# Start-up of a complex linear-attention kernel: q and k side by side in memory, the decays formed later, and TensorE summing running products of two units

## Chip, core and metric

One core of a Trainium2 chip runs the whole program in one launch. The metric is the device time of one execution in microseconds (us), as the median of several runs.

## What is computed

Inputs have batch 4, 8 heads, 768 positions and head size 48. The first layer is a linear attention with a complex gate for each position and head dimension:

```
mag = sqrt(a_re^2 + a_im^2);  scale = min(mag, 0.999) / (mag + 1e-6);  a = scale * (a_re + i a_im)
S_t = a_t * S_(t-1) + k_t v_t^T        # S: 48 x 48, complex, one per head
y_t = q_t^T Re(S_t)
```

Its output (4 x 768 x 384) goes through a feed-forward layer (384 to 1024 and back, relu, a three-tap convolution over positions, a sigmoid gate), and then through a layer of four softmax attention experts of head size 64, of which each position takes two. All of it is fp32.

## The kernel before

A batch row is a stage of its own; the four rows run one after another (`main(b)` on each engine), and during a row's later stages the gates, q and k of the next row are prepared. The order of instructions on each engine is written out by hand, with semaphores between engines: an engine never reorders, so a wait holds everything behind it.

For the recurrence a row is cut into 6 chunks of 128 positions, and each chunk into two runs of 64 from its middle. W holds the running product of the gates of each run (`w_re`, `w_im`). The preparation works on three units of two chunks each, and goes through these steps:

- gates: square, magnitude, logarithm, exponential, three DVE steps (`norm`), `write_w`.
- running products (`cum`): a run of 64 is laid out as 8 groups of 8. Steps 0 to 6 multiply along one axis and steps 7 to 9 combine the last column by doubling, for all three units at once (`HEAD` = 10 steps, four DVE instructions each). Then one `cum_fill` for each unit multiplies the inner 7 x 7 of each run by its group's factor: three products (`cum_products`: re*re, im*im, re*im), and in `cum_combine` a subtraction, the fourth product and an addition, each waiting for the one before.
- 1/|W|^2: ACT squares both parts (`w_squares`), DVE adds them (`w_sumsq`), ACT takes ln and exp (`w_ln`, `w_guess`), DVE makes a Newton step of two instructions (`inverse`).
- q and k: two DVE instructions scale half of each (`scale_qk`), four products for each chunk multiply them by W (`products_by_chunk`, L1082 and L1085). SP stores the four to `qk_dram` (`store_first_chunk` for the first chunk of a unit, `store_unit` for the second; only row 0 stores chunks apart) and loads them back with heads in place of tiles (`load_heads`).
- `decay`: twelve DVE instructions on 15 columns form what carries the state from chunk to chunk; SP stores and reloads it.

After that, for each chunk c: TensorE transposes k (`transpose_k`, L1435), ACT copies it to `ktok` (`copy_k`, L638), TensorE makes the scores (L1448), the chunk's state gain (`gain`, L1460), the rotated state (L1472) and the outputs (L1497, L1499); DVE masks the scores (`mask`, L1093), adds the gain to the state (`state_sum`, L1108 for chunk 0 and L1111 after) and steps it (`state_step`, L1126 to L1131). `copy_x` (ACT) and `x_low` (DVE) write the chunk's output for the feed-forward layer, whose first products (L1513) for the second half of the positions wait for `x_low` of chunk 5.

Row 0 has nothing to hide its preparation behind. In this start-up TensorE also forms the low part of the first weight matrix (`w_in_rest`, L1422 and L1423: twelve matmuls of 512 columns into `wide[0]` to `wide[2]`; ACT takes them out with `w_in_low`, L629) and then runs three idle matmuls (`keep_busy`, L1415), before `transpose_k(0, 0)`. One fp32 matmul of 512 columns is two MATMUL records in the trace. The rest waits for `s_r0` of unit 0:

```
            pe.wait_ge(s_r0, 1)
            ...
            for k in range(KT):
                w_in_rest(k)
            keep_busy(HOLD)
            pe.wait_ge(s_winl, 1)
            transpose_k(0, 0, 0)
```

Of the kernel before, what the change touches and what calls it, by code (L numbers as in the profile page):

```python
# [40 lines left out]
P = 128  # L41
B, H, S, D = 4, 8, 768, 48
DM = H * D
# [39 lines left out]
HOLD = 3  # L83
LAST = B - 1
# [4 lines left out]
def program(nc, a_in, qk_in, v_in, w_in, conv_w, w_out, w_q, w_k, w_vg, w_o, consts, out, g_dram, qk_dram):  # L89
    with ExitStack() as ctx:  # L90
# [82 lines left out]
        qk_slot = heads[0:2 * D, :].rearrange("p (n x h t) -> p n x h t", n=SLOTS_A, x=2, h=H)  # L173
# [100 lines left out]
        s_gl = sem("decay_loaded")  # L274
        s_wsq = sem("w_squares")
# [74 lines left out]
        def k_of(c, hd):  # L350
            return qk_slot[:, c % SLOTS_A, 1, hd, :]

        def q_of(c, hd):
            return qk_slot[:, c % SLOTS_A, 0, hd, :]
# [16 lines left out]
        def cum_count(b, k):  # L371

            return b * (HEAD * HEAD_OPS + UNITS * FILL_OPS) + min(k, HEAD) * HEAD_OPS + max(k - HEAD, 0) * FILL_OPS
# [26 lines left out]

        def cum_fill(u):
# [6 lines left out]
            return ((lambda w: groups(w)[:, t, 0:WITHIN, 1:GROUP]),  # L410
                    (lambda w: groups(w)[:, t, WITHIN:GROUP, 0:WITHIN]
                     .broadcast_to([P, UNIT_RUNS, WITHIN, WITHIN])), temps)

# [16 lines left out]
        def _(sp):  # L430
# [33 lines left out]
            def store_unit(b, u):  # L464
# [3 lines left out]
                for n, (x, part, src) in enumerate(products):  # L468
                    sp.wait_ge(s_pr, 4 * (UNITS * b + u) + n + 1)
                    skip = 1 if b == 0 else 0  # L470
                    dst = qk_dram[x, part, UNIT_CHUNKS * u + skip:UNIT_CHUNKS * (u + 1)].rearrange("c (i p) t -> p (c i) t", p=P)
                    sp.dma_start(dst, tiles(src, u)[:, KT * skip:, :]).then_inc(s_sto[u], 16)

            def store_first_chunk(u):
# [3 lines left out]
                for n, (x, part, src) in enumerate(products):  # L478
                    sp.wait_ge(s_pr0, 4 * u + n + 1)
                    c = UNIT_CHUNKS * u  # L480
                    dst = qk_dram[x, part, c:c + 1].rearrange("c (i p) t -> p (c i) t", p=P)
# [104 lines left out]
        def _(act):  # L586
# [18 lines left out]

            def w_squares(b, u):

                act.wait_ge(s_cum, cum_done(b, u))
# [4 lines left out]
            def w_ln(b, u):  # L613
                act.wait_ge(s_n, UNITS * b + u + 1)
                nc.scalar.activation(m[:, 1, unit(u)], m[:, 0, unit(u)], ACT.Ln).then_inc(s_nl, 1)
# [129 lines left out]
            def main(b):  # L745
                more = b + 1 < B
                for c in range(NC):
# [7 lines left out]
                    if b == 0:  # L755
# [5 lines left out]
                        if c == 3:  # L761
                            guess(1, 0)
# [121 lines left out]
            nc.scalar.activation(negated[:], ident[:], ACT.Copy, scale=-1.0).then_inc(s_neg, 1)  # L884
# [951 lines left out]
```

## Time and profile before

| what | value |
|---|---|
| median of 3 runs | 757.24 us (754.28 to 763.18) |
| the profiled execution's own time | 751.82 us |
| its span on the core | 749.8 us |
| TensorE busy | 662.7 us (88%) |
| VectorE (DVE) busy | 614.0 us (82%) |
| ScalarE (ACT) busy | 410.4 us (55%) |
| mean granted TensorE clock | 0.998 |

The profiled execution took 2.0 us more than its span, and it lies 5.4 us below the median of the three timed runs: differences of a few microseconds between runs are of the size of the scatter. The rows of a timeline give the start in us, the duration in us, the engine, the line, the operation, what it writes and reads, its shape and its count; in brackets stand the engine's idle time before it and who ended it.

### The profile page before, as it was taken

What the parts mean: (1) busy time and instruction counts of PE and PEld (TensorE: products, weight loads), DVE (VectorE), ACT (ScalarE), POOL (GpSimd) and SP (SyncE); (2) the same over time, 40 slices, a digit from 0 to 9 for tenths busy, and PEclk for the clock granted to TensorE, in tenths of its full rate; (3) what the DMA queues carried; (4) which work ended last, traced back from release to release, by engine and by line L of the source; (5) the groups of instructions that cost most, each with busy time, mean ns of one, the idle gap of its engine ahead of it and who ended that gap; (6) DMA issues with size and microseconds to landing.
All of it is one profiled execution on the core that took longest, in us unless ns stands there. A gap on an engine that the chain in (4) does not pass through costs nothing.

```text
span 749.8 us, 13183 instructions
## 1 busy us (share of the span) xinstructions
PE 662.7 (88%) x5226; PEld 501.4 (67%) x5226; DVE 614.0 (82%) x1165; ACT 410.4 (55%) x747; POOL 0.2 (0%) x4
## 2 busy tenths in 40 slices
PE   0006989999999999999999999999999999999998
PEld 0002768776666788776566788776566888998765
DVE  3999998999999787998989787998988675773663
ACT  6404367434667656335668647335667335654565
POOL 0000000000000000000000000000000000000000
PEclk9999999999999999999999999999999999999999
DMA  8704785200049464100058464100055440000001
GB/s 342 270 0 119 203 244 189 93 0 1 0 121 271 121 181 159 61 0 1 0 142 258 124 175 167 48 1 0 1 147 170 131 128 2 1 0 1 2 22 43
DMA packets 93628, 73.84 MB, mean 98 GB/s; under 512 B 8704, under 2 KB 85760, under 8 KB 92928
## 3 DMA queue, kind: packets, MB, share of 16 engines
q1 hardware_dynamic: 93568, 73.01, 32.1%
q8 instruction: 41, 0.67, 0.4%
q14 instruction: 19, 0.16, 0.1%
HBM read 49.34 MB, written 23.65 MB: 97 GB/s over the span
## 4 chain that ended last, share of the span: by engine, by line
PE 53%; DVE 32%; ACT 7%; issue 3%; DMA 3%; SPq 0%; DVEq 0%; ACTq 0%
DVE cv L1138 6%; PE wide L1603 6%; PE wide L1448 5%; PE wide L1584 5%; PE bank L1655 4%; PE wide L1639 4%; PE bank L1663 4%; PE wide L1460 3%; PE wide L1513 3%; DVE m L956 3%; PE wide L1534 3%; DVE heads L1143 3%; PE wide L1579 2%; DVE m L955 2%; PE wide L1575 2%
## 5 line engine op out<-in xcount | busy, mean ns | idle before, releaser
L1513 PE MATMUL wide<-x_hi_lo,win_hi 128*128 128x384 f32 x384 | 107.7, 350 | 3.4 <-DVE x_hi_lo L1102 2.6
L1513 PEld LDWEIGHTS wide<-x_hi_lo,win_hi 128*128 128x128 f32 x384 | 69.8, 188 | 7.7 <-issue 4.6
L1534 PE MATMUL wide<-heads,wout 128*128 128x384 f32 x200 | 70.1, 494 | 4.8 <-DVE heads L1143 4.8
L1202 DVE TENSOR_REDUCE nmax<-wide 128x1 f32<-128x768 f32 (+2 forms) x96 | 55.3, 618 | 21.1 <-PE wide L1613 21.0
L1138 DVE SCALAR_TENSOR_TENSOR cv<-h,wconv,cv 128x768 f32<-128x768 f32 x64 | 64.9, 1014 | 9.0 <-ACT cv L681 7.4
L1603 PE MATMUL wide<-attn 64*128 64x512 f32 (+3 forms) x256 | 65.0, 482 | 2.3 <-ACT attn L705 2.3
L1513 PE MATMUL wide<-x_hi_lo,win_lo 128*128 128x384 f32 x192 | 64.5, 336 | 0.0
L729 ACT ACTIVATE xs<-wide 128x896 f32<-128x896 f32 x48 | 44.1, 918 | 37.1 <-PE wide L1639 37.1
L655 ACT ACTIVATE h<-wide 128x384 f32<-128x384 f32 x64 | 29.6, 490 | 56.0 <-PE wide L1513 29.2
L1422 PE MATMUL wide<-attn,ident 128*128 128x512 f32 x4 | 3.9, 1082 | 62.3 <-ACT m L620 62.3
L1534 PEld LDWEIGHTS wide<-heads,wout 128*128 128x128 f32 x200 | 36.6, 189 | 30.5 <-DVE heads L1143 10.3
L686 ACT ACTIVATE cv<-cv 128x768 f32<-128x768 f32 x32 | 27.1, 846 | 48.6 <-DVE cv L1138 48.4
L1448 PE MATMUL wide<-heads 96*128 96x128 f32 x384 | 49.4, 283 | 3.8 <-DMA heads<-heads_dram 2.1
L1448 PEld LDWEIGHTS wide<-heads 96*128 96x128 f32 x384 | 45.6, 194 | 8.1 <-issue 4.1
L1655 PE MATMUL bank<-xs,attn 128*64 128x128 f32 x672 | 46.4, 279 | 0.2 <-ACT xs L729 0.2
L1655 PEld LDWEIGHTS bank<-xs,attn 128*64 128x64 f32 x672 | 35.8, 136 | 13.5 <-ACT xs L729 8.1
L1422 PEld LDWEIGHTS wide<-attn,ident 128*128 128x128 f32 x4 | 1.2, 323 | 63.3 <-issue 63.3
L1603 PEld LDWEIGHTS wide<-attn 64*128 64x128 f32 x256 | 25.5, 184 | 24.1 <-issue 9.3
L720 ACT ACTIVATE cv<-wide,nmax 128x768 f32<-128x768 f32 (+2 forms) x48 | 38.0, 792 | 2.9 <-DVE nmax L1202 2.5
L1093 DVE TENSOR_TENSOR attn<-wide,cmask 128x512 f32<-128x512 f32 x48 | 31.0, 682 | 9.6 <-PE wide L1448 9.6
L1639 PE MATMUL wide<-ident,cv 128*128 128x128 f32 x240 | 34.9, 276 | 3.5 <-DVE cv L1217 2.3
L1513 PEld LDWEIGHTS wide<-x_hi_lo,win_lo 128*128 128x128 f32 x192 | 36.1, 188 | 2.0
(205 smaller groups left out, 1505.1 us busy)
## 6 DMA issues: line engine op xcount, KB each, us to landing
heads<-heads_dram SPq DMA_DIRECT2D x96, 192.0 KB, 3.6
araw<-a_in SPq DMA_DIRECT2D x12, 768.0 KB, 6.2
araw<-qk_in SPq DMA_DIRECT2D x12, 768.0 KB, 4.7
heads_dram<-m SPq DMA_DIRECT2D x18, 384.0 KB, 3.6
heads_dram<-araw SPq DMA_DIRECT2D x18, 384.0 KB, 2.9
v<-v_in SPq DMA_DIRECT2D x4, 1536.0 KB, 6.7
out_dram<-h SPq DMA_DIRECT2D x24, 192.0 KB, 2.1
heads_dram<-m SPq DMA_DIRECT2D x12, 192.0 KB, 2.8
```

What stands on the lines that cost most here:

```text
L720: nc.scalar.activation(prob[side][:, t % 2, 0:n], slot_scores(t, side), ACT.Exp, bias=nmax[:, t, side:side + 1], accum_out=zsum[:, t, side ...
L729: nc.scalar.activation(probT[:, t % PROBT, :], wide[2][:, 0:KEYS], ACT.Copy).then_inc(s_pc, 1)
L1093: TT(sc[:, c % 2, 4 * quad:4 * quad + 4, :], low[2 + quad].rearrange("p (h t) -> p h t", h=4), cmask[:].unsqueeze(1).broadcast_to([P, 4, P ...
L1138: STT(cb, hb[:, tap:tap + S], wconv[:, mt, tap:tap + 1], cb, ALU.mult, ALU.add).then_inc(s_c, 1)
L1202: dve.tensor_reduce(nmax[:, t, side:side + 1], slot_scores(t, side), AXX, ALU.max, negate=True).then_inc(s_nm, 1)
L1448: last = MM(low[2 + quad][:, hh * P:(hh + 1) * P], k_of(c, hd), q_of(c, hd), start=True, stop=True)
L1513: last = MM(low[u % 2][:, 0:NT], w[:, k, mt * P:(mt + 1) * P], xs[:, k, n * NT:(n + 1) * NT], start=(k == 0 and part == 0), stop=(k == KT ...
L1534: last = MM(mlp_bank[u][:, 0:NT], wout[:, mt, k * P:(k + 1) * P], hgate(mt)[:, n * NT:(n + 1) * NT], start=(mt == 0), stop=(mt == MT - 1))
L1584: last = MM(bank_u[:, 0:NT], w[:, k, i * P:(i + 1) * P], xT[:, k, n * NT:(n + 1) * NT], start=(k == 0), stop=(k == KT - 1))
L1603: MM(slot_scores(t, side)[:, lo:hi], qT[rows, e // 2, i * P:(i + 1) * P], kT[rows, e // 2, lo:hi], start=True, stop=hi != keys(t, side))
L1639: last = nc.tensor.transpose(dst[:, j * P:(j + 1) * P], prob[side][:, t % 2, j * P:(j + 1) * P], ident[:])
L1655: last = MM(out_bank[side][rows, o:o + P], vx[:, j, e * HD:(e + 1) * HD], probT[:, (t + r) % PROBT, span(t, side)][:, j * P:(j + 1) * P], ...
```

## The change

Four things are changed.

1. `qk_dram` is laid out (part, chunk, row, q or k, position) in place of (q or k, part, chunk, row, position), and `heads` likewise, so that q and k of a row are 1024 bytes side by side. A `load_heads` then issues two DMAs of 384 KB in place of four of 192 KB; stores are as many as before and write runs of 512 bytes, 1024 bytes apart.
2. In row 0, units 1 and 2 are filled in another way. DVE makes all four products and no sum (`summed_product`; the fourth goes to `xs`), TensorE adds them with identity matmuls in PSUM (`fill_sums`), ACT copies the two sums into W (`fill_copy`). The sum of squares of unit 1 is also made by TensorE (`w_sums`), and read from PSUM by `w_ln` and `inverse_first`. TensorE starts `w_in_rest` after seven steps of `cum` and not after unit 0's exponential.
3. In row 0, `decay` runs right after the products of chunk 0, and its store stands before `store_unit(0, 0)` on SP.
4. In row 0, the ACT table load and `ln(1, 0)` for the next row move from behind `copy_x(0, 2)` to behind `copy_k(0, 4)`.

The order on ACT, DVE, TensorE and SP in the start-up, with the new functions (parts left out are marked):

```diff
-        qk_slot = heads[0:2 * D, :].rearrange("p (n x h t) -> p n x h t", n=SLOTS_A, x=2, h=H)
+        qk_slot = heads[0:2 * D, :].rearrange("p (n h x t) -> p n h x t", n=SLOTS_A, h=H, x=2)
...
-                for x in range(2):
-                    for part in range(2):
-                        sp.dma_start(qk_slot[part * D:(part + 1) * D, c % SLOTS_A, x, :, :],
-                                     qk_dram[x, part, c].rearrange("(h d) t -> d h t", d=D)).then_inc(s_hd[c % SLOTS_A], 16)
+                for part in range(2):
+                    sp.dma_start(qk_slot[part * D:(part + 1) * D, c % SLOTS_A].rearrange("p h x t -> p h (x t)"),
+                                 qk_dram[part, c].rearrange("(h d) x t -> d h (x t)", d=D)).then_inc(s_hd[c % SLOTS_A], 16)
...
             store_first_chunk(0)
+            store_decay(0)
             store_unit(0, 0)
             load_heads(0, 0)
             load_heads(0, 1)
-            store_decay(0)
             load_decay(0)
...
+            def fill_copy(u, part):
+                act.wait_ge(s_fm, 4 * (u - 1) + part + 3)
+                act.wait_ge(s_fs, 2 * (u - 1) + part + 1)
+                nc.scalar.activation(fill_of((w_re, w_im)[part], u),
+                                     fill_sum(part).rearrange("p n (i g) -> p n i g", g=WITHIN),
+                                     ACT.Copy).then_inc(s_fc, 1)
...
                         if c == 3:
+                            exp_tables()
+                            ln(1, 0)
                             guess(1, 0)
...
                         if c == 2:
                             magnitude(1, 1)
-                            exp_tables()
-                            ln(1, 0)
...
+            w_in_low(0)
             w_squares(0, 0)
+            w_in_low(1)
             w_ln(0, 0)
             w_guess(0, 0)
+            w_in_low(2)
+            for part in range(2):
+                fill_copy(1, part)
             w_squares(0, 1)
-            w_in_low(0)
             w_ln(0, 1)
             w_guess(0, 1)
-            w_in_low(1)
-            w_in_low(2)
+            for part in range(2):
+                fill_copy(2, part)
+            w_squares(0, 2)
             copy_k(0, 0)
-            w_squares(0, 2)
...
             cum(0, 0, HEAD + 1)
-            for u in range(2):
-                cum_products(0, HEAD + 1 + u)
-                w_sumsq(0, u)
-                cum_combine(0, HEAD + 1 + u)
-                if u == 1:
-                    decay(0)
-                inverse(0, u)
-                scale_qk(0, u)
-                products_by_chunk(u, 0)
-                if u == 1:
-                    w_sumsq(0, UNITS - 1)
-                    mask(0, 0)
-                    state_sum(0, 0)
-                products_by_chunk(u, 1)
+            for n in range(3):
+                summed_product(1, n)
+            w_sumsq(0, 0)
+            summed_product(1, 3)
+            for n in range(2):
+                summed_product(2, n)
+            inverse(0, 0)
+            scale_qk(0, 0)
+            products_by_chunk(0, 0)
+            decay(0)
+            for n in range(2, 4):
+                summed_product(2, n)
+            products_by_chunk(0, 1)
+            inverse(0, 1)
+            scale_qk(0, 1)
+            dve.wait_ge(s_fc, 2)
+            products_by_chunk(1, 0)
+            w_sumsq(0, UNITS - 1)
+            mask(0, 0)
+            state_sum(0, 0)
+            products_by_chunk(1, 1)
...
+            def fill_sums(u):
+                planes_of = ((m[:, 0, unit(u)], ident, m[:, 1, unit(u)], negated),
+                             (m[:, 2, unit(u)], ident, fill_extra(u), ident))
+                for part, (one, one_by, other, other_by) in enumerate(planes_of):
...
+                    pe.wait_ge(s_fm, 4 * (u - 1) + 2 * part + 2)
+                    for runs_of in (slice(0, GROUP), slice(GROUP, UNIT_RUNS)):
+                        cols = slice(runs_of.start * fill_size, runs_of.stop * fill_size)
+                        MM(fill_sum(part)[:, runs_of, :], one_by[:], one[:, cols], start=True, stop=False)
+                        last = MM(fill_sum(part)[:, runs_of, :], other_by[:], other[:, cols], start=False, stop=True)
+                    last.then_inc(s_fs, 1)
+            def w_sums():
+                pe.wait_ge(s_winl, KT)
+                pe.wait_ge(s_wsq, SUMMED[0] + 1)
...
-            pe.wait_ge(s_r0, 1)
+            pe.wait_ge(s_cum, cum_count(0, WITHIN))
             pe.wait_ge(s_neg, 1)
             pe.wait_ge(s_winh, KT)
             for k in range(KT):
                 w_in_rest(k)
+            fill_sums(1)
+            w_sums()
+            fill_sums(2)
             keep_busy(HOLD)
-            pe.wait_ge(s_winl, 1)
+            pe.wait_ge(s_fc, 4)
             transpose_k(0, 0, 0)
             transpose_k(0, 0, 1)
-            pe.wait_ge(s_winl, 2)
             scores(0, 0)
             pe.wait_ge(s_cast, 2)
-            pe.wait_ge(s_winl, KT)
+            pe.wait_ge(s_rn, 2 * SUMMED[0] + 1)
             gain(0, 0)
```

`fill_size` is 49, so a part of `fill_sums` has 588 columns, each multiplied twice; `w_sums` has 768 columns, each multiplied twice.

## Rows read from the trace of the kernel before

**Rows 1.** The page, part 4: the chain that ended last, by engine.

```profile
PE 53%; DVE 32%; ACT 7%; issue 3%; DMA 3%; SPq 0%; DVEq 0%; ACTq 0%
```

**Rows 2.** Busy time by stage: stretch, length, PE, PEld, DVE, ACT, POOL, PEclk, DMA, GB/s.

```profile
125.00:200.00 75.00, 72.26 (x296) 53.90 (x297) 70.53 (x117) 38.41 (x65) 0.00 (x0) 1.00 0.14 48
```

**Rows 3.** Waits for a DMA between 250 and 330 us: total, times, longest.

```profile
PEld wide L1448 <- DMA heads<-heads_dram: 0.2, 1, 0.2
```

**Rows 4.** Timeline of DVE in the start-up.

```profile
47.48 0.68 DVE L955 TENSOR_TENSOR m<-W 128x504 f32<-128x504 f32 x1
...
57.46 0.77 DVE L959 TENSOR_TENSOR m<-W 128x588 f32<-128x588 f32 x1
...
59.51 0.95 DVE L1031 TENSOR_TENSOR m<-m 128x768 f32<-128x768 f32 x1
60.38 0.77 DVE L973 TENSOR_TENSOR W<-m 128x588 f32<-128x588 f32 x1
...
62.67 0.95 DVE L1037 TENSOR_TENSOR m<-m 128x768 f32<-128x768 f32 x1
...
75.12 0.18 DVE L1008 TENSOR_TENSOR lf<-W,first 128x15 f32<-128x15 f32 x1
...
76.78 0.96 DVE L1037 TENSOR_TENSOR m<-m 128x768 f32<-128x768 f32 x1
...
84.43 1.02 DVE L1082 TENSOR_TENSOR m<-araw,W 128x384 f32<-128x384 f32 x2
...
88.62 0.55 DVE L1129 TENSOR_TENSOR st<-bank,gcol 96x384 f32<-96x384 f32 x1 [0.45 <-PE bank L1472]
...
90.47 0.55 DVE L1111 TENSOR_TENSOR attn<-wide,st 96x384 f32<-96x384 f32 x1 [0.70 <-PE wide L1460]
```

**Rows 5.** Timeline of TensorE, start-up and the scores of chunk 4.

```profile
62.32 2.04 PE L1422 MATMUL wide<-attn,ident 128*128 128x512 f32 x2 [62.32 <-ACT m L620]
...
75.29 2.74 PE L1415 MATMUL bank<-attn,ident 128*128 128x512 f32 x6
77.86 0.83 PE L1435 MATMUL wide<-ident,heads 96*128 96x96 f32 x8
...
80.34 1.48 PE L1460 MATMUL wide<-v,cv 128*96 128x48 f32 x16
...
83.60 2.84 PE L1448 MATMUL wide<-heads 96*128 96x128 f32 x16 [1.78 <-DVE attn L1093]
...
106.97 2.05 PE L1448 MATMUL wide<-heads 96*128 96x128 f32 x16 [1.13 <-DMA heads<-heads_dram]
```

**Rows 6.** Timeline of ACT in the start-up.

```profile
57.46 1.49 ACT L609 ACTIVATE m<-W 128x1536 f32<-128x1536 f32 x1 [28.98 <-DVE W L977]
...
68.62 1.03 ACT L629 ACTIVATE win_lo<-wide 128x1024 fp32r<-128x1024 f32 x1 [4.35 <-PE wide L1423]
```

**Rows 7.** Timeline of SP's queue: the loads of chunks 0 and 1, and of chunk 4.

```profile
70.86 4.21 SPq L495 DMA_DIRECT2D heads<-heads_dram  x8
...
101.61 1.87 SPq L495 DMA_DIRECT2D heads<-heads_dram  x4
```

**Rows 8.** The page, part 6: DMA issues, KB each, median us from issue to landing.

```profile
heads<-heads_dram SPq DMA_DIRECT2D x96, 192.0 KB, 3.6
...
araw<-qk_in SPq DMA_DIRECT2D x12, 768.0 KB, 4.7
```

**Rows 9.** Timeline of ACT behind chunk 2 of row 0.

```profile
109.72 1.28 ACT L625 ACT_TABLE_LOAD   x1
...
111.86 0.85 ACT L638 ACTIVATE cv<-wide 128x384 f32<-128x384 f32 x2
...
115.91 0.89 ACT L646 ACTIVATE x_hi_lo<-bank 128x192 fp32r<-128x192 f32 x2 [0.75 <-PE bank L1497]
```

**Rows 10.** Single microseconds with the granted clock (eighth column, PEclk).

```profile
85.00:86.00 1.00, 1.00 (x6) 1.00 (x6) 0.97 (x3) 0.00 (x0) 0.00 (x0) 0.50 0.09 21
...
111.00:112.00 1.00, 0.00 (x0) 0.00 (x0) 0.96 (x3) 0.99 (x3) 0.00 (x0) 1.00 0.58 175
```

More of the change, by code:

```diff
@@ L83 @@
 HOLD = 3
+SUMMED = (1, 2)
 LAST = B - 1
@@ L274, in program @@
         s_gl = sem("decay_loaded")
+        s_fm = sem("fill_products_summed_unit")
+        s_fs = sem("fill_sums")
+        s_fc = sem("fill_sums_copied")
         s_wsq = sem("w_squares")
@@ L409, in cum_fill, with fill_extra, fill_sum, w_total @@
                      for r in range(3)]
-            return ((lambda w: groups(w)[:, t, 0:WITHIN, 1:GROUP]),
+            return ((lambda w: fill_of(w, u)),
                     (lambda w: groups(w)[:, t, WITHIN:GROUP, 0:WITHIN]
                      .broadcast_to([P, UNIT_RUNS, WITHIN, WITHIN])), temps)
+        fill_size = WITHIN * WITHIN
+        def fill_extra(u):
+            return xs[:, (u - 1) * UNIT_RUNS * fill_size:u * UNIT_RUNS * fill_size]
+        def fill_sum(part):
+            return wide[part][:, 0:UNIT_RUNS * HALF].rearrange("p (n x) -> p n x", x=HALF)[:, :, 0:fill_size]
+        def w_total(b, u):
+            return wide[2][:, 0:UC] if (b, u) == (0, SUMMED[0]) else m[:, 0, unit(u)]
         def in_order(x, c, side):
@@ L604, in guess @@
                 nc.scalar.activation(m[:, 0, unit(u)], m[:, 0, unit(u)], ACT.Exp, scale=-1.0).then_inc(s_y0, 1)
+            def fill_copy(u, part):
[4 more added lines that the diff above has]
+                                     ACT.Copy).then_inc(s_fc, 1)
             def w_squares(b, u):
-                act.wait_ge(s_cum, cum_done(b, u))
+                if b == 0 and u in SUMMED:
+                    act.wait_ge(s_fc, 2 * u)
+                else:
+                    act.wait_ge(s_cum, cum_done(b, u))
                 nc.scalar.activation(m[:, 0:2, unit(u)],
@@ L614, in w_ln @@
                 act.wait_ge(s_n, UNITS * b + u + 1)
-                nc.scalar.activation(m[:, 1, unit(u)], m[:, 0, unit(u)], ACT.Ln).then_inc(s_nl, 1)
+                nc.scalar.activation(m[:, 1, unit(u)], w_total(b, u), ACT.Ln).then_inc(s_nl, 1)
             def w_guess(b, u):
@@ L944, in write_w, with summed_product @@
                    ALU.mult).then_inc(s_wn, 1)
+            def summed_product(u, n):
+                if n == 0:
+                    dve.wait_ge(s_cum, cum_count(0, HEAD))
+                val, fac, temps = cum_fill(u)
+                by = ((w_re, w_re), (w_im, w_im), (w_re, w_im), (w_im, w_re))[n]
+                dst = temps[n] if n < 3 else fill_extra(u).rearrange("p (n i g) -> p n i g", n=UNIT_RUNS, g=WITHIN)
+                TT(dst, val(by[0]), fac(by[1]), ALU.mult).then_inc(s_fm, 1)
             def cum_products(b, k):
@@ L1001, in decay @@
                 n = 12 * b
[L1002 removed]
+                dve.wait_ge(s_cum, cum_count(b, HEAD))
                 if b:
@@ L1033, in inverse_first @@
             def inverse_first(b, u):
-                total, y0, t = (m[:, r, unit(u)] for r in range(3))
+                y0, t = (m[:, r, unit(u)] for r in (1, 2))
                 dve.wait_ge(s_r0, UNITS * b + u + 1)
-                TT(t, total, y0, ALU.mult).then_inc(s_rn, 1)
+                TT(t, w_total(b, u), y0, ALU.mult).then_inc(s_rn, 1)
             def inverse_second(b, u):
@@ L1424, in w_in_rest @@
                 last.then_inc(s_wrest, 1)
+            def fill_sums(u):
+                planes_of = ((m[:, 0, unit(u)], ident, m[:, 1, unit(u)], negated),
+                             (m[:, 2, unit(u)], ident, fill_extra(u), ident))
+                for part, (one, one_by, other, other_by) in enumerate(planes_of):
+                    if u == 1:
+                        pe.wait_ge(s_winl, part + 1)
+                    else:
+                        pe.wait_ge(s_fc, 2 * (u - 2) + part + 1)
+                    pe.wait_ge(s_fm, 4 * (u - 1) + 2 * part + 2)
[7 more added lines that the diff above has]
+                pe.wait_ge(s_wsq, SUMMED[0] + 1)
+                for cols in (slice(0, 512), slice(512, UC)):
+                    for r in range(2):
+                        last = MM(w_total(0, SUMMED[0])[:, cols], ident[:], m[:, r, unit(SUMMED[0])][:, cols],
+                                  start=r == 0, stop=r == 1)
+                last.then_inc(s_n, 1)
             def transpose_k(b, c, part):
@@ L1831 @@
     g_dram = nc.dram_tensor("decay_dram", (DM, NC - 1, 2), F32, kind="Internal").ap()
-    qk_dram = nc.dram_tensor("heads_dram", (2, 2, NC, DM, CH), F32, kind="Internal").ap()
+    qk_dram = nc.dram_tensor("heads_dram", (2, NC, DM, 2, CH), F32, kind="Internal").ap()
     program(nc, *args, out, g_dram, qk_dram)
```

18 lines of the change are left out of this document (10 added, 8 removed).

## The prediction

> **What bounds the kernel now.** I read the page's chain by engine first: 53% of the span hangs on TensorE and 32% on DVE [rows 1], so stages with different limits follow each other. The stage table then says where the change can act. From 125 us on, TensorE is busy 72.26 of 75 us [rows 2], on feed-forward and attention work that the change doesn't touch; the loads it does touch hold TensorE's weight loads up by 0.2 us in the second row's whole attention stage [rows 3]. So rows 1 to 3 of the batch gain nothing from faster loads, and what counts is by how much the first feed-forward product of row 0 starts earlier: behind it everything moves along.
>
> In the start-up the DVE timeline has no idle time in brackets from 57.46 to 84.43, then waits of 0.45 and 0.70 us at 88.62 and 90.47 [rows 4]. TensorE starts at 62.32 and waits between its stages [rows 5], ACT idles 28.98 us before unit 0's squares [rows 6]. DVE alone is the limit there. After 90 us the limit changes hands: chunk 4's scores wait 1.13 us for their load [rows 5], and then ACT stands before `copy_k(0, 4)` with a table load and a logarithm [rows 9].
>
> **Part 1, DVE's own work.** Of unit 1 today, three products take 59.51 - 57.46 = 2.05 us, or 0.68 each; the subtraction, the fourth product and the addition, each waiting for the last, take 62.67 - 60.38 = 2.29 [rows 4]. After the change these become one product: -1.61 for each of two units, -3.22. The sum of squares of unit 1 goes to TensorE: 60.38 - 59.51 = 0.87 [rows 4]. Together DVE has 4.1 us less. `decay` costs 76.78 - 75.12 = 1.66 us wherever it stands [rows 4], and the rest of the list is only reordered. `inverse_first` of unit 1 reads its total from PSUM; no row shows that form, I take 0, with 0.3 us more or less as bounds from the other PSUM readers. If nothing else held DVE, the second chunk's products of unit 1 would start at 84.43 - 4.1 = 80.3.
>
> **Part 2, are the sums there in time?** TensorE may start when seven of ten steps are done, at 47.48 [rows 4]. `w_in_rest` takes 75.29 - 62.32 = 12.97 us, its slow first microseconds included, so it ends at 60.5; a 512-column fp32 matmul then costs 2.57 / 3 = 0.86 us (from 75.29 to 77.86 [rows 5]), 1.68 ns a column. One part of `fill_sums` is 1,176 columns, 1.97 us; `w_sums` is 1,536, 2.6 us. Fill sums of unit 1: 60.5 to 64.4. ACT copies the second part until about 65.1 (0.6 us each, scaled from the 1.03 us for 1,024 [rows 6]), squares for 1.49 us [rows 6] to 66.6. `w_sums` to 69.2, `w_ln` and `w_guess` at some 0.9 each to 71.0. DVE asks for it at 76.78 - 4.1 = 72.7: 1.7 us in time. Fill sums of unit 2 run from 69.2 to 73.1, `keep_busy` to 75.7; the copies and squares of unit 2 end on ACT near 75.4, before `copy_k(0, 0)` is due. The first fill copy queues behind `w_in_low(2)`, which costs nothing at this slack. So 10.5 us of new TensorE work and some 2.5 us of new ACT work lie in time that both had free. That cover is 1.7 us thick on the path through ln and guess; if it's gone, DVE waits at `inverse(0, 1)`.
>
> **Part 3, SP's queue.** This is the step that takes part of the gain back. SP must issue `store_unit(0, 0)` before it loads chunk 0. Its products come later than today: the four of them now stand behind `decay` (1.66) and two products (1.37), while the list before starts 0.24 earlier (2.05 + 0.87 + 3 x 0.68 = 4.96 against 5.21). That is +2.8 us, so the loads that start at 70.86 today [rows 7] start at 73.65. The moved decay store is one DMA, issued while SP waits for those products anyway; the decay's reload stays behind the loads of chunks 0 and 1, well before the first `state_step`, whose second instruction runs at 88.62 [rows 4]. How long does a group take from first issue to last landing? Today 106.97 - 101.61 = 5.3 us for chunk 4 [rows 5, 7]. With two issues of some 0.47 us (1.87 / 4) the lower bound is 0.5 + 3.6 = 4.1, if 384 KB land as fast as 192 KB do [rows 8]; the upper bound is today's 5.3. I take 4.9, nearer to the row of 768 KB, 4.7 us [rows 8], since the same 768 KB have to move. Chunk 0's transposes start at 78.55 and not at 77.86 [rows 5]. No row shows packets of 1024 bytes. The Trainium skill (DMA: Bandwidth & Descriptors, Specifications) puts the transfer from which the full rate is reached at 512 bytes, the size of today's packets; by it the longer ones bring no rate, and the load would stay near the upper bound.
>
> From the transposes to the end of chunk 0's gain TensorE takes 81.82 - 77.86 = 3.96 us [rows 5], so the gain is there at 82.5, `state_sum(0, 0)` follows, and the products of unit 1's second chunk start near 83.05: 1.4 earlier than 84.43, and not 4.1. DVE idles 2.7 us between. But scores of chunk 1 then start at 82.5 in place of 83.60, at full clock (today 2.84 us, against 2.05 for the same sixteen at 106.97 [rows 5]), and the waits of 0.45 and 0.70 [rows 4] go. From 90.47 on row 0 is 1.4 + 1.15 = 2.5 us early.
>
> **Part 4, chunk 4 and the moved table load.** `store_first_chunk(2)` follows DVE, so chunk 4's load starts 2.5 earlier and takes 0.4 less. `copy_k(0, 4)` no longer has 111.86 - 109.72 = 2.14 us of table load and logarithm before it [rows 9], so the gain of chunk 4 comes 4.6 earlier. That isn't kept: the same 2.14 us now stand between `copy_k(0, 4)` and `copy_x(0, 3)`, and ACT's list up to `copy_x(0, 3)` is as long as before. What is won is the 0.75 us that ACT waited there for TensorE [rows 9]. Behind it come `x_low(0, 3)`, the mask of chunk 5, the state step and the outputs, the same chain as now. Sum at the first feed-forward product: -2.5 - 0.75 = -3.2 us.
>
> The profiled execution takes 751.82 us, span 749.8 and 2.0 around it; by the sum it would take 748.6. The median of the runs is 757.24, so I forecast 754.0.
>
> **The rivals.**
> (a) More comes through. The load of chunk 0 lands at its lower bound, 0.8 us earlier, and DVE's waits close up: at most the 4.1 of part 1 and the 0.75 of part 4, some -5 us, 752.3. For it: fewer issues. Against it: SP's 2.8 us delay is arithmetic.
> (b) The load gains nothing, because packets are not 1024 bytes long or because their length doesn't matter, which is what the skill's page named above would have. Then chunk 0's transposes start at 78.95, and the sum is -2.8 us, 754.4.
> (c) TensorE's clock takes the place of DVE. Today a wait of 1.78 us before 83.60 [rows 5] is followed by a granted clock of 0.50, the 1.2 GHz level (85 to 86 us [rows 10]); a wait as long between 111 and 113 left it at 1.00 [rows 10]. After the change TensorE has a wait of about 2.2 us before `w_sums` and one of 2.8 us before the transposes of chunk 0. If those 3.96 us run mostly at the low level, some 2.5 us come on top, and the sum is -0.8, 756.4. For it: both new waits are longer than the one that was followed by a fall. Against it: one of two such waits was harmless.
> (d) It gets slower: the new work stands in TensorE's queue ahead of chunk 0's transposes. If the clock falls in the wait before `w_sums` and stays low, `w_sums`, the sums of unit 2 and `keep_busy` double from 9.1 to 18.2 us, so the transposes start at 66.6 + 18.2 = 84.8, 6.3 after 78.55. Then the sum is 6.3 - 3.2 = +3.1 us, 760.3. It decides from the point at which this work ends after 78.55 + 3.2 = 81.8. Against it: `w_in_rest` came up to full speed within its first third (68.62 - 62.32 = 6.3 us for the first of three equal parts [rows 5, 6]), and continuous work would do so again.
>
> **How the numbers follow.** Forecast 0.48 (754.0), (a) 0.12 (752.3), (b) 0.07 (754.4), (c) 0.27 (756.4), (d) 0.06 (760.3). All lie within 0.7% of 757.24; a change of 1%, 7.6 us, is about what a measurement of this kernel tells from none, with runs from 754.28 to 763.18. The median of a few such runs moves by some 3 us. From (a) less 3 to (c) plus 3 is 749.3 to 759.4; I give 749 to 759.5. Faster by over 1% (below 749.7) needs (a) or the forecast and a good draw: 0.14. Slower by over 1% (above 764.8) needs (d) and a bad one: 0.04. Within 1%: 0.82.
>
> **What would show it.** Right: no wait of DVE between 57.46 and unit 1's inverse, which starts at 72.7; sums of unit 2 done by 73.1; loads of chunk 0 issued at 73.65; a DVE wait of some 2.7 us around the mask and state sum of chunk 0; products of unit 1's second chunk at 83.05; `copy_k(0, 4)` straight behind `magnitude(1, 1)`; the first feed-forward product of the second half of the positions 3.2 us earlier than today, and the same distances after it. The decisive place is the start of chunk 0's transposes: at 77.8 or earlier it's (a), at 78.5 with slow matmuls (c), after 81 (d). Wrong in kind would be a difference that arises after 130 us, in stages of which I say that nothing changes, such as longer landings of the stores that now write runs 1024 bytes apart.

## The result and the profile after

The changed kernel takes 758.54 us (median of 20 runs), the kernel before 754.96 us (20 runs): a ratio of 1.0047, with an interval of 1.0031 to 1.0063. It is 0.5% slower where I had forecast 0.4% faster. The profiled execution took 759.44 us, the one of before 751.82; that one was a low draw, 3.1 us below its median, so the profiles lie further apart than the medians.

Up to 84 us the changed kernel runs nearly as forecast. The timeline of DVE after the change:

```profile
57.23 2.13 DVE L994 TENSOR_TENSOR m<-W 128x588 f32<-128x588 f32 x3
...
73.50 0.96 DVE L1087 TENSOR_TENSOR m<-wide,m 128x768 f32<-128x768 f32 x1 [1.10 <-ACT m L655]
...
81.24 0.69 DVE L1143 TENSOR_TENSOR attn<-wide,cmask 128x512 f32<-128x512 f32 x1 [1.58 <-PE wide L1534]
...
83.93 1.01 DVE L1132 TENSOR_TENSOR m<-araw,W 128x384 f32<-128x384 f32 x2
...
88.82 0.55 DVE L1161 TENSOR_TENSOR attn<-wide,st 96x384 f32<-96x384 f32 x1
```

The last row answers to the one that started at 90.47 in [rows 4]: DVE is 1.65 us ahead there. Then TensorE's timeline shows where that goes:

```profile
60.80 0.82 PE L1497 MATMUL wide<-m,ident 128*128 128x392 f32 x2
...
67.35 4.40 PE L1508 MATMUL wide<-m,ident 128*128 128x512 f32 x8 [2.42 <-ACT m L644]
...
79.43 0.85 PE L1521 MATMUL wide<-ident,heads 96*128 96x96 f32 x8 [1.15 <-DMA heads<-heads_dram]
...
92.58 3.78 PE L1534 MATMUL wide<-heads 96*128 96x128 f32 x16 [3.37 <-DMA heads<-heads_dram]
...
109.46 2.05 PE L1534 MATMUL wide<-heads 96*128 96x128 f32 x16 [0.69 <-DMA heads<-heads_dram]
...
118.36 3.78 PE L1534 MATMUL wide<-heads 96*128 96x128 f32 x16 [2.01 <-DMA heads<-heads_dram]
...
131.06 0.41 PE L1599 MATMUL wide<-x_hi_lo,win_hi 128*128 128x384 f32 x1 [1.38 <-DVE x_hi_lo L1152]
```

Three scores wait for their load (chunks 2, 4 and 5), the first of them 3.37 us. The last row is the first feed-forward product of the second half of the positions; the same matmul of the kernel before is its L1513:

```profile
125.53 0.42 PE L1513 MATMUL wide<-x_hi_lo,win_hi 128*128 128x384 f32 x1 [1.24 <-DVE x_hi_lo L1102]
```

So row 0 comes 5.5 us late in place of 3.2 early. Part of that is the low draw of the one profile of before: e4 and e12 below are the kernel before but for one moved step, ran near the median (755.19 and 754.79 us), and have this product at 129.23 and 129.42. Against them the changed kernel is 1.6 to 1.8 us late here. The windows of the changed kernel (columns as in [rows 2]) show that three of TensorE's waits, those of 2.42, 3.37 and 2.01 us, are followed by the low level of its clock, 1.2 GHz:

```profile
67.00:72.00 5.00, 4.65 (x10) 2.56 (x11) 4.72 (x19) 0.42 (x2) 0.00 (x0) 0.66 0.57 161
79.00:91.00 12.00, 9.78 (x114) 8.72 (x114) 9.38 (x16) 4.18 (x8) 0.00 (x0) 1.00 0.80 169
91.00:98.00 7.00, 5.42 (x26) 5.14 (x26) 5.88 (x12) 0.81 (x2) 0.00 (x0) 0.51 1.04 308
...
118.00:125.00 7.00, 6.64 (x50) 5.41 (x54) 4.27 (x8) 3.16 (x4) 0.00 (x0) 0.52 0.12 46
```

SP's queue says why chunk 2's load was late:

```profile
73.00 2.63 SPq L520 DMA_DIRECT2D heads<-heads_dram  x4
75.67 0.98 SPq L487 DMA_DIRECT2D gcol<-decay_dram  x2
77.29 1.89 SPq L508 DMA_DIRECT2D heads_dram<-m  x2
79.22 3.19 SPq L508 DMA_DIRECT2D heads_dram<-araw  x2
86.53 0.84 SPq L520 DMA_DIRECT2D heads<-heads_dram  x2
```

The loads of chunks 0 and 1 go at 73.00, later than 70.86 in [rows 7]. The decay's reload and the stores of unit 1's first chunk follow at once; four stores need 5.1 us of SP (2.2 in the kernel before, from 80.91 to 83.09), and chunk 2's load, which waits for them to land, goes at 86.53. And a load itself takes longer. Queue and issue rows of the page (parts 3 and 6):

```profile
q1 hardware_dynamic: 74368, 73.00, 33.9%
...
heads<-heads_dram SPq DMA_DIRECT2D x48, 384.0 KB, 5.5
```

Half the issues with double the bytes land in 5.5 us, against 3.6 in [rows 8]. From the first issue to the last landing of one chunk that is by these medians, as an estimate, some 0.4 + 5.5 = 5.9 us with two issues, and 1.4 + 3.6 = 5.0 with four.

### The profile page after: what moved, and what is told of

Same layout as the page of the kernel before. It is cut to its first block, busy times and chain, and to the rows that moved or that the text cites. A ratio compares the mean times of both kernels' runs of the same rounds, so it can differ in the third digit from the quotient of the medians.

```text
span 757.7 us, 13224 instructions
## 1 busy us (share of the span) xinstructions
PE 679.4 (90%) x5266; PEld 512.8 (68%) x5266; DVE 611.0 (81%) x1160; ACT 411.9 (54%) x751; POOL 0.2 (0%) x4
## 3 DMA queue, kind: packets, MB, share of 16 engines
q1 hardware_dynamic: 74368, 73.00, 33.9%
## 4 chain that ended last, share of the span: by engine, by line
PE 51%; DVE 27%; DMA 8%; ACT 8%; issue 3%; SPq 2%; DVEq 0%; ACTq 0%
DVE cv L1188 6%; PE wide L1689 5%; PE wide L1670 5%; PE wide L1534 4%; DMA heads_dram<-araw 4%; PE bank L1741 4%; PE wide L1725 3%; PE bank L1749 3%; PE wide L1599 3%; PE wide L1620 3%; DVE m L1006 3%; PE wide L1546 3%; DVE heads L1193 3%; DMA araw<-a_in 2%; PE wide L1665 2%
## 5 line engine op out<-in xcount | busy, mean ns | idle before, releaser
L1534 PE MATMUL wide<-heads 96*128 96x128 f32 x384 | 52.1, 292 | 6.5 <-DMA heads<-heads_dram 6.5
L1534 PEld LDWEIGHTS wide<-heads 96*128 96x128 f32 x384 | 48.2, 203 | 10.8 <-DMA heads<-heads_dram 7.6
L1620 PE MATMUL bank<-heads,wout 128*128 128x384 f32 x100 | 36.3, 486 | 0.0
```

The source lines that it names most:

```text
L1534: last = MM(low[2 + quad][:, hh * P:(hh + 1) * P], k_of(c, hd), q_of(c, hd), start=True, stop=True)
L1620: last = MM(mlp_bank[u][:, 0:NT], wout[:, mt, k * P:(k + 1) * P], hgate(mt)[:, n * NT:(n + 1) * NT], start=(mt == 0), stop=(mt == MT - 1))
```

## The experiments

For each kernel the ratio is to the kernel before on the same chip, with its interval; e1 to e13 have 12 runs each. It isn't the quotient of the two medians: that would be 1.0022 for e2, 0.9995 for e5 and 1.0002 for e8. So differences of under 0.2% between two rows say nothing. "Time at the low level" is worked out from each run's mean granted clock and span, as 2 x (1 - clock) x span, and is the mean over the runs; for the kernel before it is that of its 122 runs beside e1 to e13.

| kernel | median us | ratio | low level us |
|---|---|---|---|
| before (122 runs) | 755.2 | 1 | 12.2 |
| changed | 758.54 | 1.0047 (1.0031 to 1.0063) | 17.4 |
| e1 part 1 of the diff alone | 758.3 | 1.0044 (1.0021 to 1.0067) | 10.7 |
| e2 changed, old layout | 757.16 | 1.0035 (1.0012 to 1.0058) | 17.6 |
| e3 new layout, four loads, 512 bytes | 753.51 | 0.9989 (0.9968 to 1.0010) | 10.5 |
| e4 table load moved alone | 754.5 | 0.9993 (0.9973 to 1.0014) | 9.8 |
| e5 new layout, four loads, 1024 bytes | 754.73 | 0.9978 (0.9958 to 0.9998) | 9.5 |
| e6 e2, decay later | 755.76 | 1.0011 (0.9991 to 1.0032) | 12.6 |
| e7 e6, reload later too | 752.26 | 0.9963 (0.9940 to 0.9986) | 7.9 |
| e8 before, waits filled | 755.26 | 0.9984 (0.9963 to 1.0004) | 5.2 |
| e9 e7 with e5's loads | 751.04 | 0.9954 (0.9930 to 0.9978) | 8.0 |
| e10 changed, four loads | 755.58 | 1.0016 (0.9992 to 1.0041) | 16.7 |
| e11 e2, reload later | 756.28 | 1.0024 (1.0000 to 1.0049) | 15.7 |
| e12 before, reload later | 755.03 | 1.0000 (0.9975 to 1.0026) | 11.1 |
| e13 e7 with HOLD 3 | 752.42 | 0.9974 (0.9950 to 0.9999) | 8.4 |

Within one kernel's runs the time rises by 0.3 to 0.6 us for each us at the low level (0.31 over the 122 runs of before, 0.38 over those of the changed kernel).

### The layout (e1, e3, e5, e10)

e1 is the kernel before with the new layout and two loads for each chunk. e3 keeps the layout but loads as before, q and k apart in packets of 512 bytes; e5 loads packets of 1024 bytes, in four loads of 192 KB (its edit against e1, cut at the dots):

```
-                for part in range(2):
-                    sp.dma_start(qk_slot[part * D:(part + 1) * D, c % SLOTS_A].rearrange(...), qk_dram[part, c]...)
+                for half in range(2):
+                    for part in range(2):
+                        own = slice(half * H // 2, (half + 1) * H // 2)
+                        sp.dma_start(qk_slot[part * D:(part + 1) * D, c % SLOTS_A, own].rearrange(...),
+                                     qk_dram[part, c, half * DM // 2:(half + 1) * DM // 2]...)
```

> The kernel before with part 1 alone: q and k of a row side by side, two loads of 384 KB for a chunk. Theory A (the layout is what costs): the group of loads takes 6.0 to 6.6 us from first issue to last landing, against 5.3 before, and stores land later, so chunks 3 to 5 of row 0 come later and the next row's gates too, as in the changed kernel, whose rows 0 and 1 each lost 1.2 us at the last transposes of the probabilities: +3 to +6 us in all, with the first feed-forward product of the second half of row 0 at 127.5 to 129 (125.5 before) and 1.2 us lost in each of rows 0 and 1 behind it. Theory B (the crowding of SP's queue by the other parts costs, the layout is harmless): within 1 us of the kernel before, and no loss of 1.2 us in rows 0 and 1.

> The kernel before with the new layout in memory and in SBUF, but with four loads of 192 KB in runs of 512 bytes: of part 1 it keeps only the stores' runs of 512 bytes, 1024 bytes apart, and the loads' as well. If the pitch of the stores costs, the stores of the later rows land in 4 us in place of 2.9 and rows 0 and 1 lose 1.2 us each, +2.4 us or more. If only the size and the number of the loads cost, it is within 1 us of the kernel before and the groups of loads take 5.3 us as before.

> The kernel before with the new layout and packets of 1024 bytes, but four loads of 192 KB for a chunk, each with half of the heads. Theory P (a packet of 1024 bytes takes 78 ns on its DMA engine on average, against 29 for one of 512): the packets take as long as with two loads, a group of loads 6 us or more, and the kernel is as slow as with part 1 alone, +2 to +4 us. Theory S (two transfers of 384 KB land later than four of 192 KB because each is longer, whatever its packets): packets of 1024 bytes near 55 ns, groups at 5.3 us, within 1 us of the kernel before.

e1 is as slow as the whole change, with no more time at the low level than the kernel before (10.7 us); its TensorE timeline has the waits for loads, with no other part of the change in it:

```profile
94.17 2.84 PE L1447 MATMUL wide<-heads 96*128 96x128 f32 x16 [3.02 <-DMA heads<-heads_dram]
...
110.70 2.05 PE L1447 MATMUL wide<-heads 96*128 96x128 f32 x16 [1.20 <-DMA heads<-heads_dram]
...
119.23 2.05 PE L1447 MATMUL wide<-heads 96*128 96x128 f32 x16 [0.81 <-DMA heads<-heads_dram]
```

The first of them, 3.02 us, isn't chunk 2's own load alone; SP's queue in e1:

```profile
76.64 0.38 SPq L454 DMA_DIRECT2D decay_dram<-gp  x1
81.43 0.82 SPq L461 DMA_DIRECT2D gcol<-decay_dram  x2
...
87.95 0.84 SPq L494 DMA_DIRECT2D heads<-heads_dram  x2
```

The last load of chunk 1 lands 8.5 us after its issue at 72.7, at 81.2; in the kernel before it lands 5.1 us after 74.6, at 79.7. The decay's store, issued behind it at the same time in both, lets the reload go at 81.43 in place of 80.05, and chunk 2's load goes at 87.95 in place of 84.99. In e3 and e5, with short loads, the reload goes at 80.20 and 79.57 and chunk 2's load at 85.14 and 84.30. So in these profiles long loads also hold back what is issued behind them.

e3 and e5 aren't slow. So neither the stores into runs 1024 bytes apart (e3) nor the packets of 1024 bytes (e5) cost anything that shows; two transfers of 384 KB in place of four of 192 KB cost 0.55% (e1 against e3, on the same chip; the intervals don't touch). e5's rows:

```profile
q1 hardware_dynamic: 75136, 73.01, 31.7%
...
heads<-heads_dram SPq DMA_DIRECT2D x96, 192.0 KB, 3.6
```

Times 16 engines and the span, the packets took 0.317 x 16 x 753.8 = 3,823 us of engine time in e5, and by e1's row (74368 packets, 34.1% of 755.8 us) 4,124 in e1, for the same bytes in nearly the same number of packets. In the traces a packet of 1024 bytes took 78 ns on average in e1 and 62 ns in e5, so neither theory had this term right: 78 by the one and 55 by the other.

e10 makes the same edit in the changed kernel.

> The changed kernel with one edit: the two loads of 384 KB of a chunk become four of 192 KB by halves of the heads, still in packets of 1024 bytes. Whole computation. Theory (the size of one load is what made part 1 slow): the extra 1.2 us in each of rows 0 and 1 of the batch go, and the loads of chunks 1 to 5 take some 0.5 to 1 us less each, so 756 to 757.5 us, ratio 1.001 to 1.003 against the kernel before; still not faster, because the order of stores and reload is unchanged. Rival (the layout has no part in it, the order alone costs): 758.5, ratio 1.0045, as the changed kernel. Second rival (the order costs only together with the long loads): 752 to 753, ratio 0.996 to 0.998.

It falls from 1.0047 to 1.0016, as the theory said: by this pair about two thirds of what was lost is the long loads. But the intervals overlap, and e2 below, which also has four loads of 192 KB with the rest of the change, gives 1.0035, by which it would be a quarter. So the share of the long loads in the changed kernel isn't settled; it is shown in the kernel before (e1). Over the whole kernel TensorE waits 1.1 us before its scores for loads, and not 6.5 (one profile of each; page, part 5, first of e10, then of the changed kernel: busy, mean ns, idle time before and who ended it):

```profile
L1536 PE MATMUL wide<-heads 96*128 96x128 f32 x384 | 53.8, 298 | 1.1 <-DMA heads<-heads_dram 1.1
```

```profile
L1534 PE MATMUL wide<-heads 96*128 96x128 f32 x384 | 52.1, 292 | 6.5 <-DMA heads<-heads_dram 6.5
```

### The order of DVE and SP (e2, e6, e7, e11, e12, e13)

> The changed kernel with the old layout and four loads of 192 KB (parts 2, 3 and 4 alone). Theory A: what was forecast for these parts comes through: chunk 0's transposes near 78 to 79, the first feed-forward product of the second half at about 122.5 (125.5 before), -3 us against the kernel before. Theory B: the stores of unit 1's first chunk are still issued over 5 us behind the loads of chunks 0 and 1 and the decay's reload, TensorE still waits over 3 us for chunk 2 and its clock falls: 0 to +4 us.

e2, without the layout, gains nothing from 4.1 us less DVE work; it is slower than the kernel before, so the other parts cost time by themselves. e6 is e2 with the decay behind the products of chunk 1 in place of chunk 0 and with one idle matmul (`HOLD`) in place of three, and e7 moves the reload as well:

```
             products_by_chunk(0, 0)
-            decay(0)
-            for n in range(2, 4):
-                summed_product(2, n)
             products_by_chunk(0, 1)
+            decay(0)
+            for n in range(2, 4):
+                summed_product(2, n)
...
-HOLD = 3
+HOLD = 1
...
             store_first_chunk(0)
-            store_decay(0)
             store_unit(0, 0)
             load_heads(0, 0)
             load_heads(0, 1)
+            store_decay(0)
-            load_decay(0)
             store_first_chunk(1)
+            load_decay(0)
```

(e6 is this without the last move of `load_decay`.)

> The changed kernel with the old layout (parts 2 and 4), with the decay, its store and unit 2's last two products behind chunk 1's products again, and one idle matmul in place of three. If the place of the decay is what eats the gain of part 2, the loads of chunk 0 start at 70.7 again and not at 73.0, chunk 0's transposes at 76 to 77, and the median is 2 to 3 us below that of the changed kernel with the old layout, that is 1 to 2 below the kernel before. If the crowding is in the queue whatever the order (the reload of the decay waits on SP with the stores of unit 1's first chunk behind it), chunk 2 still comes late, at 91 or after, and it is within 1 us of the kernel before.

> As e6_stores_first, and the reload of the decay stands behind the stores of unit 1's first chunk on SP. If the wait for the decay's store holds those stores up, they are issued when DVE has the products, at 76 to 79 and not behind 80, and chunk 2's load starts 1 to 3 us earlier: another 1 to 2 us less than e6_stores_first. If not, no difference.

In e6 chunk 0's loads go at 70.38 and its transposes start at 76.65, as I had hoped, but chunk 2's scores come only at 90.73 and the time is that of the kernel before. e7 takes 3.5 us less than e6, more than the 1 to 2 us expected. SP's queue in e6, then in e7:

```profile
79.68 0.82 SPq L487 DMA_DIRECT2D gcol<-decay_dram  x2
80.54 1.67 SPq L508 DMA_DIRECT2D heads_dram<-m  x2
...
85.01 1.87 SPq L521 DMA_DIRECT2D heads<-heads_dram  x4
```

```profile
76.21 0.91 SPq L508 DMA_DIRECT2D heads_dram<-m  x2
...
80.68 1.63 SPq L487 DMA_DIRECT2D gcol<-decay_dram  x2
82.36 2.01 SPq L521 DMA_DIRECT2D heads<-heads_dram  x4
```

In e6 SP stands before the reload, which waits for the decay's store to land, and the stores behind it go at 80.54 though their data are there at about 76. In e7 they go at 76.21, chunk 2's load goes 2.65 us earlier, and the kernel is faster than e6 and than the kernel before. e11 and e12 make the reload's move alone, in e2 and in the kernel before; e13 is e7 with HOLD back at 3, so that against e11 only the decay, its store and two products have moved.

> Parts 2 to 4 of the change on the old layout (e2), with one edit: SP issues the decay's reload behind the stores of unit 1's first chunk in place of ahead of them; the decay stays where the change has it, behind chunk 0's products. Whole computation. Theory (the reload with its 8-byte packets crowds the stores of unit 1's first chunk): those stores start at 77.3 or earlier and land within 3 us, the load of chunk 2 is issued near 82.5 in place of 86.5, and the time falls from e2's 757.2 to some 754.5, ratio 0.998 to 1.000. Rival (the place of the decay, which makes the loads of chunk 0 later, costs): load of chunk 2 goes earlier but the time stays within 1 us of e2, ratio 1.002 to 1.004.

> The kernel before with one edit: SP issues the decay's reload behind the stores of unit 1's first chunk in place of ahead of them. DVE's, ACT's and TensorE's lists are untouched. Whole computation. Theory (what e7 won comes from DVE's shorter list, once transfers let it through; in the kernel before DVE sets the time up to 90 us and the reload is in nobody's way): ratio 0.999 to 1.001, load of chunk 2 at 84.5 to 85. Rival (e7's gain is the reload's place alone, the sums on TensorE bring nothing): ratio 0.996 to 0.998, load of chunk 2 at least 1 us earlier than 84.99.

> e7 with one edit: HOLD, the number of idle matmuls that keep TensorE busy ahead of chunk 0's transposes, back from 1 to 3. Whole computation. It stands between e11 and e7: against e11 only the decay, its store and unit 2's last two products have moved behind chunk 1's products. Theory (the decay's place, by which the loads of chunk 0 start at 70.4 or at 73.0, is what tells e11 from e7): as e7, ratio 0.996 to 0.998. Rival (the idle matmuls of e7 end at a luckier time for the clock): ratio 1.000 to 1.002, with transposes of chunk 0 later than 77.5 or with more time at the low clock than e7's mean of 7.9 us.

(The reload's packets have 40 bytes in the traces, and not 8 as I had written for e11.) e12 stays at 1.0000: so e7's gain isn't the reload's place alone. What else e7 and e13 have is parts 2 and 4 of the change, with 0.9963 and 0.9974; e4 shows no gain for part 4, so DVE's shorter list is the likely source, though no run has it alone. In e11 chunk 2's load goes at 84.29 in place of 85.32 in e2, but the time is that of e2 within the intervals: the rival held. e13 stays as fast as e7, so the idle matmuls aren't it. What is left between e11 (1.0024) and e13 (0.9974) is the decay's place; their intervals just don't touch. TensorE's timeline and the window from 79 to 92 us, first of e11, then of e13:

```profile
66.77 2.82 PE L1509 MATMUL wide<-m,ident 128*128 128x512 f32 x8 [2.42 <-ACT m L645]
...
73.39 2.74 PE L1473 MATMUL bank<-attn,ident 128*128 128x512 f32 x6
79.43 1.35 PE L1522 MATMUL wide<-ident,heads 96*128 96x96 f32 x8 [3.31 <-DMA heads<-heads_dram]
80.58 3.67 PE L1535 MATMUL wide<-heads 96*128 96x128 f32 x16
...
79.00:92.00 13.00, 12.57 (x66) 12.23 (x66) 5.65 (x10) 3.45 (x6) 0.00 (x0) 0.52 0.90 225
```

```profile
74.62 2.74 PE L1473 MATMUL bank<-attn,ident 128*128 128x512 f32 x6
77.20 0.83 PE L1522 MATMUL wide<-ident,heads 96*128 96x96 f32 x8
77.86 1.98 PE L1535 MATMUL wide<-heads 96*128 96x128 f32 x16
...
79.00:92.00 13.00, 12.06 (x143) 10.20 (x141) 11.79 (x21) 3.82 (x8) 0.00 (x0) 1.00 0.86 240
```

With the decay ahead, the loads of chunks 0 and 1 go at 73.0 and not at 70.4. TensorE then waits 3.31 us before the transposes, comes back at 1.2 GHz, and does 66 matmuls in 13 us where e13 does 143. e2 and e10 show the same wait (2.89 and 3.26 us) and the same low clock behind it (0.61 and 0.53 from 79 to 92). In the profiled run of the changed kernel the clock had fallen earlier, in `w_sums` (4.40 us, against the 2.82 us of e11's first row); the work then ended later, the wait was only 1.15 us, and the transposes ran at full speed.

These windows show how the clock can fall there, and not where the 0.5% between the medians arise. In e13's profile the clock falls later, behind a wait of 3.77 us for chunk 4's load, whose scores start at 106.40:

```profile
98.00:130.00 32.00, 26.89 (x355) 22.46 (x354) 21.88 (x44) 22.13 (x29) 0.00 (x0) 0.79 0.48 147
```

Its first feed-forward product of the second half starts at 128.95 and e11's at 129.21, so these two executions are level at the end of row 0. It is over the runs that e11 has 15.7 us at the low level and e13 8.4.

### The clock and the table load (e8, e4)

e8 fills waits of the kernel before with idle matmuls ahead of the scores of chunks 1, 3 and 4 of row 0:

```
+                for _ in range((0, 2, 0, 1, 1, 0)[c] if b == 0 else 0):
+                    MM(low[0], ident[:], mask_parts, start=True, stop=True)
                 for quad in range(2):
```

> The kernel before with idle matmuls in TensorE's waits before the scores of row 0: two for chunk 1, one each for chunks 3 and 4, 0.86 us each at full clock, into a bank that is free. Theory C (the falls of the granted clock in the start-up cost a third of their time): mean low-clock time falls from 13 us to under 8, and the median by 1 to 2 us. Rival: the idle matmuls cost what they save, or the clock falls at other places, and it is the same or up to 2 us slower.

The time at the low level falls from 12.2 to 5.2 us, by which the slope of 0.31 promises 2 us; the ratio is 0.9984 with 1 inside the interval. A gain of up to 0.4% isn't excluded, but none is shown. That the fillers stand in TensorE's queue and take a part of it back is likely, but not shown. e4 is part 4 of the prediction alone, the table load and logarithm moved behind `copy_k(0, 4)`.

> The kernel before with part 4 alone: the table load and the logarithm behind the copy of chunk 4's keys. By the prediction's step the copy comes 2.1 us earlier, the list of ACT up to the copy of chunk 3's output is as long, and 0.75 us is won: -0.3 to -0.8 us. The rival is that the whole 2.1 us come through (-2.1 us), or that the output copy of chunk 3 becomes the later one and nothing is won (0).

It gives 0.9993; the 0.75 us of the forecast are 0.1% and lie inside the interval, so this run neither shows nor denies them.

### The version that beats both (e9)

e9 has e7's order and e5's loads.

> The order of e7 (chunk 0's stores, loads of chunks 0 and 1, then the decay's store, the first-chunk stores of unit 1, then the decay's reload; decay and unit 2's last two products behind chunk 1's products), and beside it q and k side by side in memory with four loads of 192 KB by halves of the heads, as in e5. Whole computation. Theory (transfers behind the products set the start-up; short loads carry both gains): each edit alone gave some -0.3% and -0.2%, the two add, so some 751.5 us where the kernel before has 755.2, ratio 0.994 to 0.996; the scores of chunks 2 to 5 wait no longer for loads than in e7 (7.2 us in all). Rival (long packets only looked better through the draw of TensorE's clock): same as e7, 0.996 to 0.998, with the waits unchanged. Second rival (transfers now crowd each other earlier): 1.000 or above, and the loads of chunk 1 or 2 take over 6 us from first issue to scores.

```profile
L1536 PE MATMUL wide<-heads 96*128 96x128 f32 x384 | 49.1, 282 | 1.9 <-DMA heads<-heads_dram 1.9
```

```profile
124.22 0.42 PE L1601 MATMUL wide<-x_hi_lo,win_hi 128*128 128x384 f32 x1 [1.24 <-DVE x_hi_lo L1154]
```

It comes to 0.9954, 3.5 us less than the kernel before, about what I had forecast for the change itself. Its waits for loads before the scores are 1.9 us in place of e7's 7.4, but it isn't shown to be faster than e7 (0.9963): the intervals overlap almost wholly. Its profiled execution has the first feed-forward product of the second half at 124.22; e7's has it at 127.05 and e12's, a run of about the median, at 129.42.

## Why the prediction was wrong

**Part 1 of the prediction, DVE's work, held.** The three products take 2.13 us in one piece, and DVE comes to unit 1's inverse at 73.50 - 1.10 = 72.40, 4.4 us before the 76.78 of [rows 4] and close to the forecast 72.7; e7 and e13 against e12 point to its being worth having once it comes through.

**Part 2 held up to 1 us.** `inverse(0, 1)` started at 73.50 and not at 72.7, since `w_sums` ran at the low clock and DVE waited 1.10 us. The cover of 1.7 us that I had named was too thin for that. In e2, e10, e11 and e13, with `w_sums` at full speed (2.82 us), it started at 72.3 with no wait.

**Part 3 is the step that failed, in three of its terms.** First, the load groups. I took 4.9 us from the first issue to the last landing, with today's 5.3 as the upper bound. At chunk 0 it was 6.4 us, from 73.00 to the transposes at 79.43; since the loads went 0.65 us before the forecast 73.65, the error there came to 0.9 us: 79.43 against 78.55, with products of unit 1's second chunk at 83.93 against 83.05. This has nothing to do with the size of a load. e10, with four loads of 192 KB for each chunk, has the same:

```profile
72.98 3.98 SPq L522 DMA_DIRECT2D heads<-heads_dram  x8
```

```profile
79.42 1.26 PE L1523 MATMUL wide<-ident,heads 96*128 96x96 f32 x8 [3.26 <-DMA heads<-heads_dram]
```

My bound of 5.3 us came from chunk 4, whose load goes with no other chunk's behind it; chunk 0's has chunk 1's right behind. Behind chunk 0 the size does count: 5.5 us to land and not 3.6, and the stores and the reload behind a long load land later too. In the kernel before that alone costs 0.55% (e1 against e3). I had excluded a loss without a row that did so. Rival (b), that long packets bring no rate, is nearer, as e5 against e3 shows: 0.9978 and 0.9989 with overlapping intervals, 3.6 and 3.5 us to land. By the Trainium skill (DMA: Bandwidth & Descriptors, Specifications) the full rate is reached at 512 bytes; this pair agrees. But neither rule nor rival had the loss in it.

Second, I followed the 2.8 us of delay (2.1 as measured, 73.00 against 70.86) only to chunk 0's transposes. Behind those loads stand the reload and unit 1's first stores, and behind them chunk 2's load; I had written that the reload goes "well before the first `state_step`" and had not asked who stands behind it on SP. "From 90.47 on row 0 is 2.5 us early" ended at 92.58, where chunk 2's scores waited 3.37 us. e11 against e13, 0.5%, is the price of the decay's place.

Third, the clock. Rival (c) had the right wait, before the transposes, at 2.8 us, and it was 2.9 to 3.3 us in e2, e10 and e11. But I priced it at 2.5 us for the 3.96 us of chunk 0's work alone, while the clock stayed at 0.52 to 0.61 on average over 13 us. Over all runs the changed kernel has 17.4 us at the low level and the kernel before 12.2; by a slope of 0.38 those 5.2 us are 2.0 of the 3.6 us between the medians. This share is an estimate, and the runs don't order themselves by it: e1 loses 0.44% with 10.7 us at the low level, and e10 only 0.16% with 16.7. How the three terms share out the 3.6 us stays open.

**Part 4's 0.75 us** is too small for e4 to show or deny. In the changed kernel the chain didn't come that way: chunk 4 and chunk 5 waited for loads.

**After 130 us** I had said that nothing changes. The first product of the second feed-forward layer, 5.5 us late in row 0 against the one profile of before, is 6.75 us late in row 1 and 7.9 us late in row 2, as late as the end of the span. At the end of row 0 ACT's list has the squares for row 2 ahead of a copy of probabilities, and they now wait for their gates (changed kernel, timeline of ACT):

```profile
252.23 1.49 ACT L615 ACTIVATE m<-araw 128x1536 f32<-128x1536 f32 x1 [1.14 <-DMA araw<-a_in]
```

In the kernel before there is no such wait. e1 has the same two steps (2.8 us together, 2.4 in the changed kernel) and e3 none. Single profiles of e2, e5, e7, e9 and e10 lie between, with 0.5 to 1.7 us, and e6 and e11, whose loads are of 192 KB, lose most: 5.0 and 5.5 us. e11's wait at the same place:

```profile
251.78 1.48 ACT L616 ACTIVATE m<-araw 128x1536 f32<-128x1536 f32 x1 [2.54 <-DMA araw<-a_in]
```

So the long loads aren't the only cause of this term. It makes up 5.4 of the 5.7 us between the profiles of e11 and e13, and what sets it stays open. The prediction had named a difference behind 130 us as a sign of being wrong in kind. [Rows 3] had misled me: the loads that TensorE waits for aren't the only ones in SP's queue.

## What to carry to other kernels

When a change delays one step in a DMA queue, follow the queue to its next waiting load and not only to the first reader: here a load of chunk 0 that goes 2.6 us later decided whether 4 us less work on DVE is a gain, and moving the decay and two products behind the work that the loads wait for turned 1.0024 into 0.9974. Halving the number of transfers is no gain by itself: here a load twice as large landed 1.9 us later, so count issue and landing together. On a start-up with waits of 2 to 3 us, price a new wait of TensorE with the time at the low clock that follows it, and judge by several runs, since the one profile of the kernel before lay 3.1 us below the median.

## What the runs showed of the hardware

Two loads of 384 KB landed in 5.5 us each and four of 192 KB in 3.6, and the kernel with the long ones used 8% more engine time for the same bytes in packets of the same length (4,124 us in e1 against 3,823 in e5; 78 against 62 ns for a packet of 1024 bytes). I had expected equal engine time and have no cause for it. The granted clock fell after waits of 2.4 us (`w_sums`) in the changed kernel's profile and didn't fall after the same 2.42 us in that of e11, so that two executions with the same order of work on TensorE up to there differ.
